# Attention start-up on one core: two bias tables move to GpSimd, one PSUM copy changes place, and TensorE's filler products start earlier and last longer

## The reference, cut to what matters

```python
# attention: B, H, S, D = 2, 8, 768, 64; a key is kept if it is one of the first n_global = 8
# or at most n_local - 1 = 95 positions back
scores = q @ k.T / sqrt(D) + bias            # bias = -slope[h] * distance, slope[h] = 2 ** -(h + 1)
scores = where(keep, scores, -1e9)
a = exp(scores - max(scores)); a = a / (sum(a) + 1e-9)
x = a @ v                                     # then heads side by side: [2, 768, 512]
# first block:  u = x + (x.T @ U @ V).T;  x = u + relu(u @ w_ch1) @ w_ch2
# second block: h = relu(x @ w_in), two halves, one normalised and mixed over tokens by w_spatial,
#               out = (u * v_s) @ w_out
```

## Time and profile before

| | us |
|---|---|
| median of 3 runs | 495.59 (495.51 to 495.88) |
| the profiled execution, its own time | 498.07 |
| its span, first to last instruction | 496.3 |
| busy: PE, DVE, ACT, POOL | 491.2, 311.0, 222.6, 249.0 |
| mean granted TensorE clock by the profile | 0.999 |

### The profile page before, as it was taken

How to read it: one execution, slowest core, us unless ns; L and a number is a source line. 1 busy time by engine, 2 the same in 40 slices (tenths; PEclk the granted TensorE clock), 3 DMA queues, 4 the chain that set the end, 5 groups by cost and what they waited for, 6 DMA issues and landing times.

```text
span 496.3 us, 7920 instructions
## 1 busy us (share of the span) xinstructions
PE 491.2 (99%) x2786; PEld 411.1 (83%) x2786; DVE 311.0 (63%) x726; ACT 222.6 (45%) x521; POOL 249.0 (50%) x219
## 2 busy tenths in 40 slices
PE   8999999999999999999999999999999999999997
PEld 8888777887888888888888888888888889998985
DVE  4888788521259465564665646547868888878600
ACT  7788889632235533341332422415452356333121
POOL 6698567353335776845476456132885201950000
PEclk9999999999999999999999999999999999999999
DMA  8541701123222421122221120220113000001022
GB/s 236 203 155 65 238 2 44 45 85 96 75 87 89 166 85 32 54 85 86 71 100 37 49 85 0 87 63 2 63 65 114 4 0 1 1 1 43 22 89 102
DMA packets 14552, 36.27 MB, mean 73 GB/s; under 512 B 2480, under 2 KB 2480, under 8 KB 14512
## 3 DMA queue, kind: packets, MB, share of 16 engines
q1 hardware_dynamic: 12640, 32.35, 19.3%
q10 hardware_dynamic: 1872, 3.41, 1.8%
HBM read 32.61 MB, written 3.15 MB: 72 GB/s over the span
## 4 chain that ended last, share of the span: by engine, by line
PE 98%; DVE 1%; issue 0%; ACT 0%; POOL 0%; POOLq 0%; ACTq 0%
PE bank L1755 15%; PE bank L1481 13%; PE bank L1687 9%; PE bank L1612 9%; PE bank L1784 9%; PE bank L1777 9%; PE bank L1837 8%; PE bank L1855 7%; PE bank L1537 5%; PE bank L1519 5%; PE bank L1504 5%; PE bank L1473 2%; PE bank L1551 1%; PE bank L1559 1%; PE bank L1584 1%; PE bank L1573 1%
## 5 line engine op out<-in xcount | busy, mean ns | idle before, releaser
L520 POOL TENSOR_TENSOR w_slot<-stage,w_slot 128x1024 fp32r<-128x1024 f32 x30 | 73.2, 2449 | 65.1 <-ACT w_slot L1227 65.1
L918 DVE TENSOR_TENSOR uT<-bank,uT 128x512 f32<-128x512 f32 x68 | 45.8, 689 | 25.3 <-PE bank L1784 23.2
L1157 ACT ACTIVATE prob<-prob,row_min 128x256 f32<-128x256 f32 (+1 forms) x96 | 45.9, 480 | 9.3 <-DVE row_min L736 9.2
L1755 PE MATMUL bank<-u_op,s_slot 128*128 128x512 f32 x192 | 47.6, 389 | 0.0
L1687 PE MATMUL bank<-hid,w_slot 128*128 128x512 f32 x192 | 46.9, 393 | 0.0
L1612 PE MATMUL bank<-u_split,w_slot 128*128 128x512 f32 x192 | 46.5, 391 | 0.0
L1777 PE MATMUL bank<-hid,w_slot 128*128 128x512 f32 x192 | 46.1, 389 | 0.0
L1784 PE MATMUL bank<-hid,w_slot 128*128 128x512 f32 x192 | 46.1, 389 | 0.0
L956 DVE TENSOR_TENSOR part<-part,bank 128x512 f32<-128x512 f32 x40 | 27.4, 685 | 26.8 <-PE bank L1755 26.4
L1687 PEld LDWEIGHTS bank<-hid,w_slot 128*128 128x128 f32 x192 | 35.7, 188 | 8.2 <-issue 0.9
L1755 PEld LDWEIGHTS bank<-u_op,s_slot 128*128 128x128 f32 x192 | 36.0, 188 | 7.5
(11 more groups left out here) (149 smaller groups left out, 965.0 us busy)
## 6 DMA issues: line engine op xcount, KB each, us to landing
stage<-in_w_ch SPq DMA_DIRECT2D x32, 512.0 KB, 3.3
qk_raw<-in_qk SPq DMA_DIRECT2D x23, 256.0 KB, 4.9
v_all<-in_v SPq DMA_DIRECT2D x12, 256.0 KB, 5.2
out_dram<-o_stage ACTq DMA_DIRECT2D x12, 256.0 KB, 2.0
stage<-in_w_spT SPq DMA_DIRECT2D x6, 384.0 KB, 3.0
stage<-in_w_in SPq DMA_DIRECT2D x4, 512.0 KB, 4.3
stage<-in_w_out SPq DMA_DIRECT2D x2, 512.0 KB, 4.0
V_raw<-in_V SPq DMA_DIRECT2D x4, 96.0 KB, 4.7
```

Source lines behind the costliest of these rows:

```text
L520: nc.gpsimd.tensor_tensor(dst[:, LO, :], stage[n % 2][:, 0:w], dst[:, HI, :].bitcast(F32), ALU.subtract).then_inc(w_lo, 1)
L918: vec.tensor_tensor(y, y_bank(e)[:], y, ALU.add).then_inc(y_sum, 1)
L1157: last = sc.activation(prob[r][:, e, 0:w], prob[r][:, e, 0:w], ACT.Exp, bias=row_min[:, k:k + 1], scale=-1.0, accum_out=row_sum[:, q:q + 1])
L1755: last = mm(seven_bank[held][:], lhs, u_op[op][:, m, k, :], start=not more and k == 0 and p == 0, stop=k == 1 and p == 2, skip_group_check ...
```

## The change

Five edits. A tile idle of 128x128 ones is set by DVE as its first instruction, and all fillers multiply it instead of the identity; PE's first fillers wait for it and not for the identity. Ahead of step -2, PE gets three more fillers: two behind a wait for the first rounded half of q and k (qk0_hi), one behind a wait for the distance table (dist0_set). The bias tables of heads 4 to 7 are made by GpSimd with tensor_scalar, two behind the splitting of group 3 and two behind that of group 4, and no more by ACT in step 0; GpSimd waits for dist0_set ahead of its first splitting, and score_bias(3) waits for the new semaphore bias_far. ACT runs take_probT(2) ahead of both parts of exps(3). DVE takes its part of take_probT(2) in step 1, between take_oT(1) and the second part of score_bias(3), and no more at the start of step 2.

```diff
+        idle = at("idle", [P, P], F32, SLOT * 15 + 2048 * 3)
...
+            def set_bias(first):
+
+                for h in range(first, first + 2):
+                    nc.gpsimd.tensor_scalar(bias[:, h, :], dist[:], -(2.0 ** -(h + 1)) / SCALE, None,
+                                            ALU.mult).then_inc(bias_far, 1)
...
             with pool.If(near):
+                pool.wait_ge(dist0_set, 1)
                 for g in range(2, 6):
                     split_qk(g)
+                    if g in (3, 4):
+                        set_bias(2 * g - 2)
...
+            vec.memset(idle[:], 1.0).then_inc(idle_set, 1)
             vec.memset(var_one[:], 1.0)
...
-                    elif g < 4:
+                    elif g == 2:
                         dve.wait_ge(bias_set, heads(g, m)[1][1] + 1)
+                    elif g == 3:
+                        dve.wait_ge(bias_far, heads(g, m)[1][1] + 1 - H // 2)
...
-                    if 0 <= s < QUADS:
+                    if 0 <= s < QUADS and s != 2:
                         take_probT(s)
...
                         score_bias(s + 2, 0)
                         take_oT(s)
+                        if s == 1:
+                            take_probT(2)
                         score_bias(s + 2, 1)
...
-                    if s == 0:
-                        set_bias(4)
-                        set_bias(6)
...
                     if s == 1:
-                        exps(3, 0)
                         take_probT(2)
-                        exps(3, 1)
+                        exps(3)
...
+            pe.wait_ge(idle_set, 1)
             def fill(count):
 
                 for _ in range(count):
-                    mm(aux[:, 0:P], ident[:], ident[:], start=True, stop=True)
+                    mm(aux[:, 0:P], idle[:], idle[:], start=True, stop=True)
 
-            fill(WARM)
+            fill(10)
             pe.wait_ge(ident_set, 2)
...
             with pe.If(near):
+
+                pe.wait_ge(qk0_hi, 1)
+                fill(2)
+                pe.wait_ge(dist0_set, 1)
+                fill(1)
                 for s in range(-2, QUADS):
```

More of the change, by code:

```diff
@@ L23 @@
 MASK_FILL = 1.0e9
-WARM = 10
 def build(nc, qk, qT, kT, v, cfg, U, V, w_ch, w_in, w_spT, b_sp, w_out, x_dram, out):
@@ L186, in build @@
         z_some, z_copy = sem("z_some"), sem("z_copy")
-        dist0_set, bias0_set = sem("dist0_set"), sem("bias0_set")
+        dist0_set, bias0_set, bias_far = sem("dist0_set"), sem("bias0_set"), sem("bias_far")
         bias_set, iotas, ident_set, V_split = sem("bias_set"), sem("iotas"), sem("ident_set"), sem("V_split")
+        idle_set = sem("idle_set")
         qk_in = [[sem(f"qk_in{r}_{hq}") for hq in range(2)] for r in range(3)]
@@ L1468, in _ @@
             mm = nc.tensor.matmul
-            pe.wait_ge(ident_set, 2)
+            pe.wait_ge(idle_set, 1)
             def fill(count):
                 for _ in range(count):
-                    mm(aux[:, 0:P], ident[:], ident[:], start=True, stop=True)
-            fill(WARM)
+                    mm(aux[:, 0:P], idle[:], idle[:], start=True, stop=True)
+            fill(10)
+            pe.wait_ge(ident_set, 2)
             def product(out_ap, terms):
```

## The result

| | before | after |
|---|---|---|
| median | 495.62 us (8 runs, 495.44 to 495.91) | 497.41 us (8 runs, 497.13 to 498.96) |
| profiled execution | 498.07, span 496.3 | 498.96, span 497.2 |

The ratio is 1.0037, with an interval of 1.0022 to 1.0052: the change costs 1.8 us. 493.0 was forecast, with a range that ended at 496.0.

A forecast was written before the change was run, and what follows sets the result against it. TensorE's schedule was taken as the bound, with turn(2) at 15.05 instead of 17.67 us. Early clock rise and tables off ACT, with 0.6 us of fillers inside, net 2.6 us: 495.59 to 493.0, range 492.4 to 496.0.

The forecast's parts named there:

- The bound: TensorE is the chain for 98%; a shift made before turn(2) at 17.67 us is carried to the end.
- Fillers: Start-up on TensorE: start at 1.05, scores at 6.8; 0.6 us cost by themselves, but an early clock rise, taken at 7.5.
- A: The forecast: clock rises between about 5.5 and 8.7 us, 2.3 to 2.9 us off, 492.7 to 493.3; chance 0.38.
- the crux: Sign at turn(0): transposes at 273 ns and not 421, showing the early clock rise.
- The base: Starting time: the runs' median, 2.48 us under the profiled execution, carried over: 495.59 less 2.6 us gives 493.0.
- Rival C: Timed runs of before already rise early; ACT's tables and 0.6 us of fillers left, 1.0 off, 494.6; chance 0.18.
- Tables off ACT: Ahead of exps(2) on ACT: four tables gone, worth up to 1.3 us, only beside the early clock rise.
- Tables on GpSimd: Ahead of copy_k(4): four tables at 0.40 us, 1.6 us in all; barely covered, 0.8 us lost at the upper bound.
- E: Slower: clock rises a step later, about 17.7 us; in all about 2.1 us lost, 497.7; chance 0.11.
- Cover at weigh(7): copy_v(7) ends 1.0 us ahead of weigh(7); GpSimd follows PE's scores and idles until 27 us, so it moves with PE.
- Group 2's copies: ACT's copy delays exps(3)'s first part about 1.2 us, still ahead of turn(3); DVE's only changes place; both nothing.
- The warning about GpSimd: Skill page implies dearer tables on GpSimd; ACT's 0.33 us against 0.40 taken as a small price, nothing while covered.

The follow-up runs named there:

- again_before: The kernel before, unedited, run again for a second trace and the spread: median 495.71 us, ratio 0.9999.
- again_after: The changed kernel, unedited, run again for a second trace and the spread: median 498.88 us, ratio 1.0052 to the kernel before.
- only_fillers: The kernel before with the change's fillers alone (idle tile, earlier start, three more ahead of step -2): 495.66 us, ratio 0.9995.
- no_tables: The kernel before with the new fillers and the tables of heads 4 to 7 made by nobody (wrong output): 495.02 us, ratio 0.9972.
- one_pair_first: The kernel before with new fillers, tables of heads 4 and 5 on GpSimd, copy_k(4) ahead of the splitting of group 5: 495.06 us, ratio 0.9987.
- copy_first: The changed kernel with copy_k(4) right behind GpSimd's second pair of tables, ahead of the splitting of group 5: 496.06 us, ratio 1.0003 to before.
- undo_tables: The changed kernel with the tables of heads 4 to 7 back on ACT in step 0: 496.00 us, ratio 0.9999 to the kernel before.
- dve_late_copies: The changed kernel with the four tables on DVE, behind score_bias(1) and ahead of score_bias(2)'s first part: 497.20 us, ratio 1.0026 to before.
- half_tables: The changed kernel with each GpSimd table made in two instructions of 128x128 instead of one of 128x256: 499.86 us, one run.
- dve_tables: The changed kernel with the four tables on DVE, two ahead of score_bias(0), two behind score_bias(1): 496.85 us, ratio 1.0024 to before.
- dve_late: The kernel before with new fillers and tables on DVE, behind score_bias(1) and ahead of score_bias(2)'s first part: 496.78 us, ratio 1.0023.
- psum_tables: The kernel before with new fillers and the tables on DVE, read from a PSUM copy of the distance table: 495.93 us, ratio 1.0001.

## Why the prediction was wrong, by its steps

**The bound.** That TensorE's schedule carries a shift to the end holds: from scores(4) on the steps are 3.46 us in again_before and in again_after, and 18.51 against 16.74 at scores(4) is the 1.8 us of the result.

**Fillers.** Start 1.05 and scores 6.74 as forecast (1.05 and 6.8). The rise came at about 6.3 us, within the range of A, but in again_after at about 4.1, where the prediction had bounded it by "not before the end of the first fillers, about 5.5". What they were to bring, an early rise, the kernel before has with its old fillers and a pause of 0.17 us in its second trace. By themselves they change the median by nothing (only_fillers). The sign that the prediction called the crux, transposes of turn(0) at 273 ns, came true and told nothing, as before shows it as well.

**The base.** The step "The median of the runs stands 2.48 us under it, and I carry the difference over" is the first that failed. That difference was the late rise of one execution: scores(4) start at 16.74 in before's usual execution and not at 19.16. That is, before's timed runs already had 2.4 of the forecast 2.6 us. Rival C named this and gave 1.0 us as the gain left; no_tables and one_pair_first measured 0.7.

**Tables off ACT.** Right as a mechanism: exps(2) started at 12.38 and turn(2) at 14.48. Mis-sized in worth, up to 1.3 against 0.7.

**Tables on GpSimd.** This is the second step that failed, and the one that made it slower. "I take 0.40, the one-input pass over the same 256 elements", with 0.64 as upper bound, measured 0.85. The four cost 3.4 us and not 1.6, the last splitting ends at 18.1 instead of 16.0, and what was "Covered, barely" became a wait of 2.40 us: scores(4) were forecast at 16.5 and came at 18.5, 2.0 us later. With the 2.4 us of the base this makes the 4.4 us between 493.0 and 497.4. The place was right, the splittings and copy_k(4) queued behind the tables; the price was wrong by twice, and the cover had been reckoned to 0.2 us. As a rival with its own price and switching point it was missing: the slower side was given to the clock (E), which did not happen that way. The clock did cost time in some executions, but by falling after the wait.

**Cover at weigh(7).** Held in the changed kernel, as PE was late itself; copy_first shows it used up, 0.62 us.

**Group 2's copies.** Priced at nothing; by the medians they cost 0.2 us alone, 0.3 in undo_tables and 0.4 in dve_late_copies, with a wait of 0.21 to 0.22 us for ACT's copy of group 3 in each trace. Each is small beside its interval, but they agree. So this step failed too, by little.

**The warning about GpSimd.** The Trainium skill (GPSIMD Engine Reference, the introduction) calls GpSimd the wrong choice for elementwise arithmetic, with VectorE roughly twice as fast. The prediction put it aside by a comparison of ACT's measured 0.33 us with my own 0.40. Measured, a table costs GpSimd 0.85 us, 2.6 times what it costs ACT, and DVE took 0.28 (its fastest) and 0.42 (from PSUM) for the same, so these traces agree with the page.

## What to carry to other kernels

When work moves to an engine that feeds the critical one, list what is queued behind it and price the moved instruction by a row of the same kind on that engine; where there is none, even the dearest rate that the engine shows can be too low (here 0.64 us against 0.85), so ask whether the cover survives twice your own price, or time the instruction first. A switch of 0.2 us of cover is a coin toss and belongs among the rivals. And before a gain is reckoned from one trace, ask whether the trace's time is that of the timed runs: here the 2.5 us between them were about as much as the whole forecast gain.

## What the runs showed of the hardware that was not expected

- GpSimd's tensor_scalar in fp32 takes 0.54 us for 128 elements a partition and 0.85 for 256 (half_tables, after): 2.4 ns an element and 0.23 us fixed. That is no cheaper an element than its two-input subtraction (1.28 us for 512), and its cast of 512 takes 0.61.
- DVE's tensor_scalar of 128x256 took from 0.28 to 1.29 us beside a busy GpSimd (dve_tables, dve_late), and 0.41 to 0.43 with its source in PSUM (psum_tables).
- Behind 2.4 us of idle TensorE the clock fell to 1.2 GHz for 3.4 us in some executions (2 of 8, then 4 of 6, and 3 of 7 with the tables alone), at 1.5 us each, and in none of ten with fillers in their place. Waits of 0.48 and 1.30 us ahead of a fall are in the trace of dve_late_copies. The fall began about 1.5 us after the work had started again in the changed kernel (20.0 against 18.48), and at once in dve_late_copies. Three executions of before have a clock of 0.997 too, at about 496.7, and stay unexplained.
- The clock's rise at the start moves between executions of one kernel: about 4.1 and 6.3 us in two traces of the changed kernel (where the filler records go from 421 to 275 ns), about 7 and 14.3 in two of the one before. All but the last were early enough to cost nothing that the start of scores(4) shows.
